# VectorE's order inside a slot: the denominator's product between the two steps of the polynomial, the spectrum's negated half behind the rounded quotient

## The reference, cut to what matters

```python
X = np.fft.rfft(x, axis=1)                       # x: 4 x 3008 x 256
Yr = Xr @ w_r - Xi @ w_i + b_r
Yi = Xr @ w_i + Xi @ w_r + b_i
Y  = soft_threshold(Yr, 0.01) + 1j * soft_threshold(Yi, 0.01)
y  = np.fft.irfft(Y, n=3008, axis=1)             # 12032 tokens of 256
h  = y @ w_in                                    # 12032 x 2048
P  = a[0] + a[1]*h + a[2]*h**2 + a[3]*h**3
Q  = 1.0 + abs(b[0])*abs(h) + abs(b[1])*h**2
out = (P / (Q + 1e-06)) @ w_out                  # 12032 x 256
```

## Time and profile before

| what | value |
|---|---|
| time, median of 3 runs | 1425.1 us (1424.39 to 1425.21) |
| span of the profiled execution | 1422.2 us |
| TensorE busy | 1381.5 us, 97% |
| VectorE busy | 1331.7 us, 94% |
| ScalarE busy | 1243.0 us, 87% |
| GpSimd busy | 632.6 us, 44% |

### The profile page before, as it was taken

How to read it: one execution, slowest core, us unless ns; L and a number is a source line. 1 busy time by engine, 2 the same in 40 slices (tenths; PEclk the granted TensorE clock), 3 DMA queues, 4 the chain that set the end, 5 groups by cost and what they waited for, 6 DMA issues and landing times.

```text
span 1422.2 us, 21592 instructions
## 1 busy us (share of the span) xinstructions
PE 1381.5 (97%) x7498; PEld 972.5 (68%) x7498; DVE 1331.7 (94%) x1639; ACT 1243.0 (87%) x1654; POOL 632.6 (44%) x417
## 2 busy tenths in 40 slices
PE   7998999999999999999999999999999999999987
PEld 3875677777767677677777776776766666666666
DVE  5687999999999999999999999999999999999998
ACT  4577999998888998988989988988889999999986
POOL 0001544444444444444445445444445555555554
PEclk9999999999999999999999999999999999999999
DMA  8976756656556656555555555565455545555443
GB/s 280 289 234 143 169 130 146 152 133 137 119 136 138 143 138 133 127 117 122 108 130 113 129 115 126 108 137 115 95 115 112 109 89 116 109 118 109 85 95 71
DMA packets 97913, 188.07 MB, mean 132 GB/s; under 512 B 11216, under 2 KB 57744, under 8 KB 97808
## 3 DMA queue, kind: packets, MB, share of 16 engines
q0 software_dynamic: 29952, 98.58, 37.5%
q1 hardware_dynamic: 67856, 88.12, 20.8%
HBM read 50.60 MB, written 37.49 MB: 62 GB/s over the span
## 4 chain that ended last, share of the span: by engine, by line
PE 66%; DVE 19%; ACT 6%; issue 6%; DMA 2%; POOL 1%; SPq 0%; ACTq 0%; POOLq 0%
PE h_ps L564 23%; PE o_ps L594 8%; PE o_ps L579 8%; PE o_ps L581 8%; DVE den L1092 4%; DVE num L1098 4%; DVE num L1112 4%; DVE g_hi L1087 4%; PE d L541 3%; PE d L505 3%; PE d L481 2%; PE d L475 2%; ACT sq L791 1%; POOL g_lo L1175 1%; ACT num L794 1%
## 5 line engine op out<-in xcount | busy, mean ns | idle before, releaser
L1175 POOL TENSOR_TENSOR g_lo<-num,sq 128x940 fp32r<-128x940 f32 (+1 forms) x205 | 471.0, 2297 | 91.4 <-DVE num L1098 90.8
L1167 POOL DMA_DIRECT2D den<-sq x208 | 182.5, 877 | 685.7 <-ACT sq L791 382.1
L579 PE MATMUL o_ps<-g_hi,wout_hi 128*128 128x470 f32 (+1 forms) x832 | 342.4, 412 | 0.9 <-DVE g_hi L1087 0.9
L581 PE MATMUL o_ps<-g_hi,wout_lo 128*128 128x470 f32 (+1 forms) x832 | 310.7, 374 | 0.0
L564 PE MATMUL h_ps<-yt_hi,win_hi 128*128 128x470 f16 (+1 forms) x832 | 301.4, 362 | 4.7 <-DVE num L1115 4.7
L564 PE MATMUL h_ps<-yt_lo,win_hi 128*128 128x470 f16 (+1 forms) x832 | 299.4, 360 | 0.0
L564 PE MATMUL h_ps<-yt_hi,win_lo 128*128 128x470 f16 (+1 forms) x832 | 299.4, 360 | 0.0
L1112 DVE TENSOR_TENSOR num<-h_ps,num 128x940 f32<-128x940 f32 (+1 forms) x208 | 232.1, 1116 | 27.8 <-ACT num L794 26.9
L1115 DVE SCALAR_TENSOR_TENSOR num<-num,coef,h_ps 128x940 f32<-128x940 f32 (+1 forms) x208 | 245.1, 1179 | 7.4
L1092 DVE SCALAR_TENSOR_TENSOR den<-den,g_hi 128x940 f32<-128x940 f32 (+1 forms) x208 | 244.2, 1174 | 0.2
L1087 DVE SCALAR_TENSOR_TENSOR g_hi<-num,a_sb,sq 128x940 fp32r<-128x940 f32 (+1 forms) x208 | 244.3, 1174 | 0.0
(11 more groups left out here) (167 smaller groups left out, 1571.3 us busy)
## 6 DMA issues: line engine op xcount, KB each, us to landing
den<-sq POOLq DMA_DIRECT2D x200, 470.0 KB, 4.4
z_in<-spec SPq DMA_DIRECT2D x96, 128.0 KB, 2.9
spec<-s_out SPq DMA_DIRECT2D x96, 128.0 KB, 2.8
xw<-in_x SPq DMA_DIRECT2D x31, 384.0 KB, 4.8
out_t<-o_sb SPq DMA_DIRECT2D x25, 470.0 KB, 4.6
spec<-s1w SPq DMA_DIRECT2D x56, 192.0 KB, 3.0
zp_in<-spec SPq DMA_DIRECT2D x22, 480.0 KB, 5.0
inv_in<-in_inv SPq DMA_DIRECT2D x96, 64.0 KB, 2.3
```

The source lines that it names most:

```text
L579: pe.matmul(o_ps[:, h, 0:w], wout_hi[:, f, h * P:(h + 1) * P], g_hi[q % 3][:, j, 0:w], start=f == 0, stop=False)
L581: mm = pe.matmul(o_ps[:, h, 0:w], wout_lo[:, f, h * P:(h + 1) * P], g_hi[q % 3][:, j, 0:w], start=False, stop=False)
L1175: pool.tensor_tensor(g_lo[r % 2][:, :, 0:cols(r)], ring(num, r), ring(sq, r), ALU.mult).then_inc(n_g, 1)
```

## The change

`lower_x` is cut in two; its second instruction becomes `negate_x`. In the slots with a chunk `negate_x` is issued after `rounded(q-1)` instead of before it. Ahead of slot 0 and in slot 0 the order stays. And `multiplied(q-2)`, which stood after the second polynomial step (and after the rare measuring steps), now stands between the first and the second.

```diff
                 dve.scalar_tensor_tensor(out=xt[c % 2][:, 1, :, 64:192], in0=both, scalar=x_scale[:, c // K2:c // K2 + 1],
                                          in1=xt[c % 2][:, 0, :, 64:192], op0=ALU.mult, op1=ALU.subtract).then_inc(e2l, 1)
+
+            def negate_x(c):
                 dve.wait_ge(e2l, c + 1)
                 dve.tensor_scalar(xt[c % 2][:, :, :, 0:64], xt[c % 2][:, :, :, 128:192], -1.0, None, ALU.mult).then_inc(e2n, 1)
...
                     dve.tensor_tensor(top, h, top, ALU.mult).then_inc(n_n2, 1)
+                if 0 <= q - 2 < NS and late(q - 2):
+                    multiplied(q - 2)
                 if q < NS:
                     dve.wait_ge(n_n2, q + 1)
                     dve.scalar_tensor_tensor(out=top, in0=top, scalar=scales(q // SLOTS, 1), in1=h,
...
-                if 0 <= q - 2 < NS and late(q - 2):
-                    multiplied(q - 2)
...
                 if q - 1 in S2_AT and q >= 2:
                     lower_x(S2_AT[q - 1], d0[:, :])
                 if 0 <= q - 1 < NS:
                     rounded(q - 1)
+                if q - 1 in S2_AT and q >= 2:
+                    negate_x(S2_AT[q - 1])
```

More of the change, by code:

```diff
@@ L1053, in _ @@
             lower_x(0, h_ps[0][:, 0, :])
+            negate_x(0)
             for u in range(1, PRE + 1):
@@ L1056, in _ @@
                     lower_x(u, h_ps[0][:, u % 2, :])
+                    negate_x(u)
                 if u == W_AT + 11:
@@ L1131, in _ @@
                     lower_x(PRE, d0[:, :])
+                    negate_x(PRE)
                     sum_abs(2 * S1N)
```

## The result

The changed kernel takes 1558.1 us (median; 1556.0 to 1559.6, 4 runs) against 1424.9 us for the kernel before (median of 4). The ratio is 1.093 with an interval of 1.0918 to 1.0943: 9.3% slower. The prediction said 1567 us, in a range of 1540 to 1605.

What follows compares the result with a forecast made beforehand. TensorE was taken to set the pace while chunks last, VectorE from slot 141; after the change VectorE everywhere. Waits of +216.7 and +4 less savings and filled idle time gave +141.7: 1422.2 to 1563.9, median 1567 us, range 1540 to 1605.

Steps and rivals of the forecast that it cites:

- The wait for the product's end: Denominator's product on VectorE ends 1.00 us after GpSimd's product; wide slots grow 1.10 us, 197 of them +216.7 us.
- the one extension in the sum: Denominator's product: wait needed is 1.21 us a slot, the longest in the trace 0.92; the last 0.29 us is extrapolated.
- a wait of a fixed, capped size: Rival, denominator's product: wait paid once at a capped 0.92 us, 37 us less, 1530 us; chance 5%.
- The longer products: Rival: GpSimd's product takes 2.51 us in each slot, 59 us more, 1626 us; chance 4%.
- The wait shortened by `soft`: Slots behind a soft one: product released before L974, so the wait is 0.34 us shorter, 67 times, -22.8 us.
- The 0.11 of the negated half: VectorE, chunk slots: parting L959 and L962 wins 0.11 us in each of 66 slots, -7.3 us.
- the negated half's later arrival: TensorE gets it some 1 us later, behind L564's twelve matmuls: costs nothing, at most 1 us in each of 66 slots.
- VectorE's idle time filled: VectorE becomes the bound everywhere and its idle time goes: 36.6 us less 5.6 before slot 0, -31.0 us.
- The bound in the early tiles: Early tiles: VectorE needs 56.5 us a tile against TensorE's 54.6, so VectorE becomes the bound, narrowly.
- No collision: Rival: VectorE and GpSimd run beside one another in the new place; 1420.8 us, 0.3% faster; chance 4%.
- No saving at all: Rival: no collision, but the first step's follower starts after 1.17 us in any case; 1427.9 us; chance 2%.
- The clock: Rival: TensorE's late work is spread out and it loses its clock; 136 us more, about 1700 us; chance 2%.

Runs made afterwards that it cites:

- half_after: The changed kernel with GpSimd's product over one of its two blocks only (470 columns), from the third product on: 1425.5 us.
- mul_only: The kernel before with only the denominator's product moved between the two steps, the negated half staying directly behind lower_x: 1565.4 us, ratio 1.0985.
- neg_only: The kernel before with only the negated half moved behind the rounded quotient: 1424.1 us, ratio 0.9991.
- the memset: The changed kernel with GpSimd's product replaced, from the third on, by a memset of the same 940 columns, which reads nothing: 1412.1 us.
- split_after: The changed kernel with GpSimd's product issued as two instructions of 470 columns each: 1509.7 us, ratio 1.0583.

## Why the prediction was right

*The wait for the product's end.* Right. L1096 ends 0.99 us after the product in the late slot above, and 0.99 to 1.01 in 197 wide slots; predicted was 1.00. A late slot takes 6.62 us for 6.64, and the chain runs over VectorE and its held instruction for 91% of the span, so VectorE is the bound, as predicted. That the wait goes past the 0.92 us which the trace before showed was the one extension in the sum, and it held (2.32 less 1.13 is 1.19). So the rival with a wait of a fixed, capped size is out; `half_after` had put such a fee at 1550 us and took 1425.5. The longer products are out too: GpSimd's group on the page has a mean of 2.18 us. The prediction took the 2.51 us of the earlier trace rows as a length that any product might have. The trace before shows what goes with it: the 107 products with an idle stretch of over 0.15 us behind GpSimd's DMA issue take 2.2 us each, and of the 96 that follow it directly 74 take 2.4 to 2.6. In the changed order nearly all have such a stretch (1.90 us in the late slot above).

*The smaller terms.* The wait shortened by `soft` was put at 0.34 and is 0.32. The 0.11 of the negated half is there: L959 and L964 take 0.54 together, and `mul_only`, without it, is 7.3 us slower. That the negated half's later arrival costs TensorE nothing was argued from the cover of L564, and `neg_only` bears it out. VectorE's idle time filled as assumed: 6.7 us are left before the first step, 5.6 of them the wait before slot 0.

*The bound in the early tiles.* Right, and as narrow as put: 56.2 us for the 56.5 predicted, with TensorE's need at 54.6. The middle tile takes 55.7, the late one 52.9 (8 x 6.64 would be 53.1).

*The size.* The sum gave +141.7, the spans differ by 132.0. The sum is so 7% too large. A slot is 0.02 us shorter than assumed in late tiles, and a pair of chunk slots without L1046 takes 13.74 (6.81 in the rows above and, from 7.54 less 0.61 for L1046, 6.93), 0.08 less than the assumed 2 x 6.64 + 0.54 = 13.82. The timeline has 34 pairs with no other small operation in them, and 30 of these take 13.71 to 13.77. Over 67 pairs and 59 late slots that makes 6 to 7 us. The other 3 us probably lie in the terms for idle time and were not separated.

*The rivals.* No collision was put at 1421 us. With the collision taken away by a shorter product the changed order does win, 5.4 us against the old order with the same product where this rival had 4.3, so its reckoning of the edit was fair and only its premise failed. No saving at all is out too: the follower of the first step starts 1.05 us after it. The clock stayed at its upper level of 2.4 GHz in the tile windows above (1.00), with TensorE busy for 43.2 of 52.9 us in the late one; that rival is out too.

The Trainium skill's rule in "SBUF — State Buffer", section "Who interferes with whom", that the pair of ports is held for a whole instruction and that a GpSimd instruction which only writes does not contend with two SBUF inputs of VectorE, agrees with the runs: L1096 ends 0.99 us after products of 1.2 and 2.2 us, and has 1.13 us beside the memset. It doesn't explain the slots of `split_after` in which L1096's record starts before the second half's and L1096 still waits for it. In "VectorE: DVE Perf Modes", the section "The DRAIN you can't avoid" says that the next operation doesn't start until the pipeline is empty, with a semaphore between or not, and also that a next operation which is not held starts earlier. The prediction's rival used the first alone. The trace here agrees with the second: 1.17 us from start to start with the dependence, 1.05 without.

## What to carry to other kernels

Before an instruction of VectorE with two tensors in SBUF is moved, look at what GpSimd does at its new start time: if it is running a product of two tensors in SBUF, nearly the whole rest of it is added (here 1.19 us of the 1.33 that were left), and the record only looks like a slow instruction. In this kernel the places that cover GpSimd's product are those with an operand in PSUM; two of them in a row, 2.28 us, cover a product of 2.21, and the 0.12 us of dependence between them is the price of that cover. And 0.11 us saved in 66 slots were worth some 7 us or about 1 us, depending on which engine set the pace.

## What was not expected of the hardware

Cutting GpSimd's product made also the old order 9 us faster (0.9936), more than the expected span; its L1092 went from a mean of 1.185 us to 1.131, which over 200 slots is 11 us of held time that was there all along. Whether the 9 us come from it was not separated, since TensorE's waiting for the product falls from 18.0 us to 3.0 as well. A product that follows GpSimd's DMA issue without an idle stretch is mostly recorded some 0.3 us longer; why is open. When two GpSimd instructions follow one another, VectorE sometimes gets in between (1.31 us) and sometimes waits for both (2.65 us).
